# Expert tiles: the hidden rows transposed in 32 by 32 blocks by VectorE and two transfers, in place of TensorE

## The chip, the cores and the metric

The kernel runs on one core of a Trainium2 chip. The number to judge is the time on the device in microseconds, from the start to the end of one execution. TensorE (PE) multiplies matrices, VectorE (DVE), ScalarE (ACT) and GpSimd (POOL) work elementwise, and SyncE (SP) mostly issues transfers. Each engine runs its own list of instructions in order. They meet at semaphores: one engine counts up, another waits for a number.

## The reference

Three layers behind each other, all in fp32: windowed attention, a gated MLP, and a layer of eight experts of which each token uses two. The change lies in the third:

```python
x: (2304, 512)   w1: (8, 512, 1024)   w2: (8, 1024, 512)
top2, top2_w = ...                      # two experts for each token, and their weights
for e in range(E):
    for k in range(2):
        mask = top2[:, k] == e
        h = np.maximum(x[mask] @ w1[e], 0.0)
        out[mask] += top2_w[mask, k, None] * (h @ w2[e])
```

## The kernel before

Tokens are sorted by expert into tiles of 128 rows, `ETILES` = 43 of them; an expert has about five tiles, and the last one or two of the 43 are padding. Products are made in three passes from operands split in two: a high part in TensorE's fp32r format and a low part, the value less the high part (`PRODUCTS`).

One tile t goes through these steps. `load_rows` (SP) brings `x_row`, already with its 32 by 32 blocks moved into place, so that `dve_xT` (VectorE) has only to transpose within blocks (L1801), and then splits the result into `xTh` and `xTl`. `pe_up2` (TensorE) makes x @ w1 in two halves of 512 columns, 12 matmuls each, in banks 0 and 1. `dve_relu` (L1834) writes max(., 0) to `relu` [128 rows, 1024]. `pe_hT` (L1075) transposes `relu` with eight transposes of 128 by 128 into banks 2 and 3. `dve_hT` splits these banks into `hTh` (L1822) and `hTl` (L1824, the bank less `hTh`). `pe_down2` (L1062) makes h @ w2 in 24 matmuls, again in two halves. `dve_y` (L1841) copies the bank to `y_row`, and `store_rows` (SP, L576) stores it; `load_rows` issues at L571.

TensorE's order in the loop is, for tile t: `pe_hT` of t-1, `pe_up2` of t, `pe_down2` of t-1. VectorE's is `dve_hT` of t-1, `dve_relu` of t, `dve_xT` of t+1, `dve_y` of t-1. `hTh`, `hTl` and `relu` exist once; semaphores guard them (`hT_done`, `hTl_done`, `relu_done`, `tile_done`).

Beside that the weights of the next expert but one arrive in 512 KB pieces on ScalarE's queue as soon as an expert's last tile is done. ScalarE casts the high part, and GpSimd makes the low part from two SBUF operands, in two TENSOR_TENSORs of 512 elements for a piece (`expert_piece_low`, L732), eight pieces for an expert. For the last expert's tiles GpSimd gathers finished rows (L750) and adds them (L763), ScalarE scales them, and a last step on VectorE (L1899) follows the last `dve_y`.

## Time and profile before

| | us |
|---|---|
| median of 3 runs | 1078.38 |
| lowest, highest | 1077.81, 1081.57 |
| the profiled execution's own time | 1076.49 |
| its span, on which all rows stand | 1074.7 |
| TensorE busy in it | 1062.6 |
| VectorE busy | 588.3 |
| ScalarE, GpSimd busy | 327.8, 386.8 |

Times in the rows are microseconds from the span's start unless marked ns. A row of a timeline has the start, the length, the engine, the line, the operation, what is written <- what is read, and how many of a kind follow each other (xN, as one length); in brackets stands how long the engine had been idle and what released it. SPq is SP's queue of transfers. A matmul's own length overlaps its neighbours', so the pace is read from starts.

### The profile page before, as it was taken

The page shows a single profiled execution, that of the slowest core. Times are in us where ns is not written, and L with a number is a line of the kernel's source. Part 1 is how long each engine was busy: PE and PEld are TensorE (multiplying, and loading weights), DVE is VectorE, ACT ScalarE, POOL GpSimd, SP SyncE. Part 2 cuts the span into 40 slices and gives each one's busy share as a digit, 9 for nine tenths or more (in the row PEclk, how much of TensorE's full clock was granted, in tenths as well). Part 3 has the DMA queues.
Part 4 walks back from the last instruction along what each step waited for, and adds up shares of the span by engine and source line. Part 5 has one row for each costly group of instructions (what it writes and reads, how often), then busy time and mean ns, then how long its engine had stood idle before and what let it go on. Part 6 is the DMA issues. An engine that isn't in the chain of part 4 may idle for free.

```text
span 1074.7 us, 20097 instructions
## 1 busy us (share of the span) xinstructions
PE 1062.6 (99%) x6053; PEld 931.9 (87%) x6054; DVE 588.3 (55%) x1226; ACT 327.8 (31%) x724; POOL 386.8 (36%) x358
## 2 busy tenths in 40 slices
PE   8999999999999999999999999999999999999998
PEld 7878999999999999999988888888888888888886
DVE  6887434363363463453447775565555556555554
ACT  7987122342342432432352111020302021110222
POOL 4667990030030030120185415070706143250486
PEclk9999999999999999999999999999999999999999
DMA  7985525411311311211074536172616344331676
GB/s 218 276 264 190 176 89 187 127 59 30 118 59 30 117 59 30 98 59 30 26 250 153 161 80 174 39 207 46 195 47 161 85 117 127 82 104 39 168 242 235
DMA packets 199634, 133.18 MB, mean 124 GB/s; under 512 B 128752, under 2 KB 161408, under 8 KB 199584
## 3 DMA queue, kind: packets, MB, share of 16 engines
q1 hardware_dynamic: 177728, 75.14, 25.9%
q10 hardware_dynamic: 16032, 38.47, 10.9%
q0 software_dynamic: 5824, 18.95, 5.1%
q8 instruction: 25, 0.41, 0.2%
q14 instruction: 25, 0.20, 0.1%
HBM read 85.87 MB, written 42.73 MB: 120 GB/s over the span
## 4 chain that ended last, share of the span: by engine, by line
PE 93%; POOL 2%; DMA 2%; issue 1%; DVE 1%; SPq 0%; POOLq 0%; ACT 0%; DVEq 0%
PE bank L873 28%; PE bank L1041 20%; PE bank L1062 20%; PE bank L905 14%; PE bank L1075 3%; PE bank L817 2%; PE bank L844 2%; PE bank L827 1%; POOL token_rows_a L750 1%; PE bank L811 1%; DMA token_rows_b<-expert_rows,slots_u 1%; PE bank L958 1%; DMA q_sb<-in_qT 1%; POOL token_rows_a L763 1%; DMA k_sb<-in_kT 0%
## 5 line engine op out<-in xcount | busy, mean ns | idle before, releaser
L873 PE MATMUL bank<-x_parts,mlp_weights 128*128 128x384 f32 x1704 | 309.4, 336 | 0.0
L873 PEld LDWEIGHTS bank<-x_parts,mlp_weights 128*128 128x128 f32 x1704 | 298.3, 188 | 5.3
L1041 PE MATMUL bank<-expert_parts,xT_high 128*128 (+1 forms) x688 | 216.6, 396 | 0.0
L1062 PE MATMUL bank<-expert_parts,hT_high 128*128 (+1 forms) x688 | 212.2, 390 | 0.0
L732 POOL TENSOR_TENSOR expert_parts<-raw_expert_a,expert_parts 128x512 fp32r<-128x512 f32 x64 | 81.4, 1305 | 234.3 <-ACT expert_parts L1372 232.0
L905 PE MATMUL bank<-mlp_weights,hidden_parts 128*128 128x512 f32 x648 | 162.1, 395 | 0.0
L1062 PEld LDWEIGHTS bank<-expert_parts,hT_high 128*128 128x128 f32 x688 | 129.0, 188 | 26.9 <-issue 0.4
L1041 PEld LDWEIGHTS bank<-expert_parts,xT_high 128*128 128x128 f32 x688 | 125.8, 188 | 24.3 <-issue 0.4
L905 PEld LDWEIGHTS bank<-mlp_weights,hidden_parts 128*128 128x128 f32 x648 | 120.2, 188 | 23.4 <-issue 1.0
L1041 PE MATMUL bank<-expert_parts,xT_low 128*128 (+1 forms) x344 | 134.4, 391 | 0.0
L1062 PE MATMUL bank<-expert_parts,hT_low 128*128 (+1 forms) x344 | 134.2, 390 | 0.0
L1565 DVE TENSOR_TENSOR hidden<-bank,sigmoid 128x384 f32<-128x384 f32 x72 | 40.1, 557 | 139.1 <-ACT sigmoid L1274 138.0
L1372 ACT CAST expert_parts<-raw_expert_a 128x1024 fp32r<-128x1024 f32 x32 | 33.5, 1049 | 262.9 <-PE bank L1062 242.3
L674 POOL TENSOR_TENSOR squares<-squares 128x384 f32<-128x384 f32 x15 | 15.1, 1008 | 251.4 <-ACT squares L1249 251.4
L1834 DVE TENSOR_SCALAR relu<-bank 128x512 f32<-128x512 f32 x86 | 59.0, 690 | 84.0 <-PE bank L1041 84.0
L1841 DVE COPY y_row<-bank 128x512 f32<-128x512 f32 x43 | 29.7, 691 | 108.0 <-PE bank L1062 108.0
L1285 ACT CAST hidden_parts<-hidden 128x384 fp32r<-128x384 f32 x72 | 36.9, 513 | 160.8 <-DVE hidden L1568 154.1
L732 POOL TENSOR_TENSOR expert_parts<-raw_expert_b,expert_parts 128x512 fp32r<-128x512 f32 x64 | 81.1, 1301 | 2.3 <-ACT expert_parts L1372 2.3
L1041 PEld LDWEIGHTS bank<-expert_parts,xT_low 128*128 128x128 f32 x344 | 64.6, 188 | 13.9
L1062 PEld LDWEIGHTS bank<-expert_parts,hT_low 128*128 128x128 f32 x344 | 64.6, 188 | 13.4
L1274 ACT ACTIVATE sigmoid<-bank 128x384 f32<-128x384 f32 x72 | 35.3, 491 | 131.6 <-PE bank L873 130.3
L1571 DVE TENSOR_TENSOR hidden_parts<-hidden,hidden_parts 128x384 fp32r<-128x384 f32 x72 | 47.3, 657 | 46.1 <-ACT hidden_parts L1285 46.1
(220 smaller groups left out, 1230.1 us busy)
## 6 DMA issues: line engine op xcount, KB each, us to landing
raw_expert_a<-in_w ACTq DMA_DIRECT2D x32, 512.0 KB, 4.6
raw_expert_b<-in_w ACTq DMA_DIRECT2D x32, 512.0 KB, 4.2
x_row<-routed_rows SPq DMA_DIRECT2D x172, 64.0 KB, 2.6
expert_rows<-y_row SPq DMA_DIRECT2D x43, 256.0 KB, 2.0
expert_rows<-zeros SPq DMA_DIRECT2D x4, 2304.0 KB, 11.9
v_sb<-in_v SPq DMA_DIRECT2D x32, 256.0 KB, 3.9
q_sb<-in_qT SPq DMA_DIRECT2D x15, 288.0 KB, 3.7
k_sb<-in_kT SPq DMA_DIRECT2D x15, 288.0 KB, 4.1
```

The costliest lines, as they stand in the source:

```text
L732: nc.gpsimd.tensor_tensor(ew_sb[:, slot, 2 * kind + 1, at:at + 512], raw_exp(q)[:, half * 512:half * 512 + 512], ew_sb[:, slot, 2 * kind, ...
L873: last = nc.tensor.matmul(bank[:, 0:CHUNK], w_sb[:, i, wp, at:at + P], xp[:, par, part, k, :], start=n == 0, stop=n == 3 * KB - 1)
L905: last = nc.tensor.matmul(ps[3 + t][:, 0:D], hp[:, i % 2, part, t * P:(t + 1) * P], w_sb[:, i, wp, 2 * KB * P:COLS], start=i == 0 and n == ...
L1041: last = nc.tensor.matmul(ps[half][:, 0:512], (xTh, xTl)[xp][:, buf, k, :], ew_sb[:, bass.ds(slot, 1), wp, k * F2 + half * 512:k * F2 + ha ...
L1062: last = nc.tensor.matmul(y_bank(t)[:, 0:D], (hTh, hTl)[hp][:, f, :], ew_sb[:, bass.ds(slot, 1), 2 + wp, f * D:(f + 1) * D].rearrange("p a ...
L1075: last = nc.tensor.transpose(ps[2 + b][:, f * P:(f + 1) * P], relu[:, col:col + P], ident[:])
L1274: nc.scalar.activation(sig[:], ps[2 * i % 3][:, 0:CHUNK], ACT.Sigmoid).then_inc(sig_done, 1)
L1285: nc.scalar.copy(hp[:, i % 2, 0], h_sb[:]).then_inc(hh_done, 1)
L1372: nc.scalar.copy(ew_sb[:, slot, 2 * kind, piece * 1024:piece * 1024 + 1024], raw_exp(q)).then_inc(expert_high, 1)
L1565: nc.vector.tensor_tensor(h_sb[:], ps[2 * i % 3][:, 0:CHUNK], sig[:], ALU.mult).then_inc(gated, 1)
L1571: nc.vector.tensor_tensor(hp[:, i % 2, 1], h_sb[:], hp[:, i % 2, 0].bitcast(F32), ALU.subtract).then_inc(hl_done, 1)
L1834: nc.vector.tensor_scalar(relu[:, half * 512:half * 512 + 512], ps[half][:], 0.0, None, ALU.max).then_inc(relu_done, 1)
```

## The change

For tiles 4 to 41 the hidden rows are no more transposed by TensorE. VectorE transposes the 32 by 32 blocks straight out of the banks of the layer up (`dve_turn`, to a new buffer `hB`), half by half. SP stores each half to DRAM and loads it back in four pieces with the blocks exchanged, into `relu` (`move_hidden`), each half as soon as it can. `dve_hidden` then takes max(., 0) and splits: the high part in one instruction, the low part in four, all from SBUF. `hB` lies in staging space that is free by then. The last tile and tiles 0 to 3 keep the old way.

```diff
+            def move_hidden(t):
+                for half in range(2):
+                    sp.wait_ge(relu_done, 2 * t + half + 1)
+                    sp.dma_start(hs_dram[t % 2, :, half * 512:half * 512 + 512], hB[:, half * 512:half * 512 + 512]
+                                 ).then_inc(hidden_out[half], 16)
+                for half in range(2):
+                    sp.wait_ge(hidden_out[half], 16 * (t + 1 - FIRST_TURNED))
+
+                    sp.wait_ge(hTl_done, 2 * t - 1 + half)
+                    blocks = hs_dram[t % 2, :, half * 512:half * 512 + 512].rearrange("(s r) (q n) -> q r s n", s=BLOCKS, q=BLOCKS)
+                    for q in range(BLOCKS):
+                        sp.dma_start(relu[q * BLOCK:(q + 1) * BLOCK, half * 512:half * 512 + 512].rearrange(
+                            "r (s n) -> r s n", s=BLOCKS), blocks[q]).then_inc(hidden_in[half], 16)
+
+            for t in range(FIRST_TURNED, ETILES - 3):
+                move_hidden(t)
+                load_rows(t + 3, (t + 3) % 2)
+                store_rows(t - 1)
...
                 now = entries(t)
                 before = entries(t - 1)
-                pe_hT(pe, t - 1)
                 pe_up2(pe, t, buf, *now)
                 pe_down2(pe, t - 1, *before)
...
+        def dve_turn(dve, t, half):
+
+            dve.wait_ge(up_done, 2 * t + half + 1)
+            if not (isinstance(t, int) and t == FIRST_TURNED):
+
+                dve.wait_ge(hidden_out[half], 16 * (t - FIRST_TURNED))
+            nc.vector.transpose(hB[:, half * 512:half * 512 + 512].rearrange("p (q f c) -> p q f c", q=BLOCKS, c=BLOCK),
+                                ps[half][:].rearrange("p (f q c) -> p q f c", q=BLOCKS, c=BLOCK)
+                                ).then_inc(relu_done, 1)
+
+        def dve_hidden(dve, t, halves=(0, 1)):
+
+            dve.wait_ge(tile_done, t)
+            for b in halves:
+                dve.wait_ge(hidden_in[b], 16 * BLOCKS * (t + 1 - FIRST_TURNED))
+                landed = relu[:, b * 512:b * 512 + 512].rearrange("p (s f c) -> p f s c", s=BLOCKS, c=BLOCK)
+                h = hTh[:, 4 * b:4 * b + 4, :].rearrange("p f (s c) -> p f s c", c=BLOCK)
+                nc.vector.tensor_scalar(h, landed, 0.0, None, ALU.max).then_inc(hTh_done, 1)
+                dve.wait_ge(hTh_done, 2 * t + b + 1)
+                low = hTl[:, 4 * b:4 * b + 4, :].rearrange("p f (s c) -> p f s c", c=BLOCK)
+                for s in range(BLOCKS):
+                    last = nc.vector.scalar_tensor_tensor(out=low[:, :, s], in0=landed[:, :, s], scalar=0.0,
+                                                          in1=h[:, :, s].bitcast(F32), op0=ALU.max,
+                                                          op1=ALU.subtract)
+                last.then_inc(hTl_done, 1)
...
             def tile(t, buf, earlier):
-                dve_hT(dve, t - 1)
-                dve_relu(dve, t)
+                dve_turn(dve, t, 0)
+                dve_hidden(dve, t - 1, (0,))
+                dve_turn(dve, t, 1)
+                dve_hidden(dve, t - 1, (1,))
                 dve_xT(dve, t + 1, buf, earlier)
                 dve_y(dve, t - 1)
```

TensorE, where one pass of the loop ends and the next tile begins (L391 and L384 read table entries for the tile, L1064 and L1032 open the layer up). Before:

```order
L1126 COMPARE_AND_BRANCH
L384 TENSOR_LOAD tab
L384 ISA x2
L1075 MATMUL bank<-ident,relu 128x128 [waits hTl_done,relu_done]
L1075 MATMUL bank<-ident,relu 128x128 x3
L1075 MATMUL bank<-ident,relu 128x128 [waits relu_done]
L1075 MATMUL bank<-ident,relu 128x128 x3
L1032 ISA [waits xTl_done]
```

The same place with the change:

```order
L1156 COMPARE_AND_BRANCH
L391 TENSOR_LOAD tab
L391 ISA x2
L1064 ISA [waits xTl_done]
```

The eight transposes are gone and the layer up of the next tile follows at once on the layer down.

VectorE, one tile of its loop. Before:

```order
L1822 CAST hT_high<-bank 128x512 [waits tile_done,hT_done]
L1824 TENSOR_TENSOR hT_low<-bank,hT_high 128x512 [waits hTh_done]
L1834 TENSOR_SCALAR relu<-bank 128x512 [waits hT_done]
L1834 TENSOR_SCALAR relu<-bank 128x512 [waits hT_done,up_done]
L1801 STREAM_TRANSPOSE bank<-x_row 128x512 [waits xTl_done,x_row_in_even]
L1809 CAST xT_high<-bank 128x512 [waits xT_done]
```

With the change (`hidden_blocks` is `hB`; L1876 is `dve_turn`, L1887 and L1891 are `dve_hidden`):

```order
L1876 STREAM_TRANSPOSE hidden_blocks<-bank 128x512 [waits hidden_out_0]
L1887 TENSOR_SCALAR hT_high<-relu 128x512 [waits hidden_in_0]
L1891 SCALAR_TENSOR_TENSOR hT_low<-relu,hT_high 128x4x32 [waits hTh_done]
L1891 SCALAR_TENSOR_TENSOR hT_low<-relu,hT_high 128x4x32 x3
L1876 STREAM_TRANSPOSE hidden_blocks<-bank 128x512 [waits hidden_out_1,up_done]
L1887 TENSOR_SCALAR hT_high<-relu 128x512 [waits hidden_in_1,tile_done]
L1831 STREAM_TRANSPOSE bank<-x_row 128x512 [waits xTl_done,x_row_in_even]
L1839 CAST xT_high<-bank 128x512 [waits xT_done]
```

The split of the tile in front no longer comes ahead of both halves of the layer up. Each half of it stands behind the transpose of a half that the layer up has to finish first.

SP's queue, one tile. Before:

```order
L384 TENSOR_LOAD tab
L571 DMA x_row<-routed_rows 32x16x32
L576 ISA [waits y_row_done]
L576 DMA expert_rows<-y_row 128x512
```

With the change:

```order
L608 DMA hidden_by_blocks<-hidden_blocks 128x512 [waits relu_done] x2
L616 DMA relu<-hidden_by_blocks 32x4x128 [waits hTl_done,hidden_out_0]
L616 DMA relu<-hidden_by_blocks 32x4x128 x3
L616 DMA relu<-hidden_by_blocks 32x4x128 [waits hTl_done,hidden_out_1]
L616 DMA relu<-hidden_by_blocks 32x4x128 x3
L391 TENSOR_LOAD tab [waits xT_done]
L581 DMA x_row<-routed_rows 32x16x32
L586 DMA expert_rows<-y_row 128x512 [waits y_row_done]
```

Ten transfers stand ahead of the load of `x_row`, and the store of `y_row` comes behind them.

## Rows read from the trace of the kernel before

**Rows 1.** The page's busy line, then TensorE's waits: total, times, longest

```profile
PE 1062.6 (99%) x6053; PEld 931.9 (87%) x6054; DVE 588.3 (55%) x1226; ACT 327.8 (31%) x724; POOL 386.8 (36%) x358
...
PE bank L1145 <- DVE ones L1907: 1.3, 1, 1.3
```

**Rows 2.** Timeline of one expert tile: start, length, engine, line

```profile
803.41 1.04 PE L1075 MATMUL bank<-ident,relu 128*128 128x128 f32 x8
...
804.21 0.70 PE L1041 MATMUL bank<-expert_parts,xT_high 128*128 x2
...
804.60 0.36 SPq L576 DMA_DIRECT2D expert_rows<-y_row  x1
...
806.62 3.06 SPq L571 DMA_DIRECT2D x_row<-routed_rows  x4
...
807.35 0.69 DVE L1834 TENSOR_SCALAR relu<-bank 128x512 f32<-128x512 f32 x1 [0.29 <-PE bank L1041]
...
809.55 0.41 PEld L1062 LDWEIGHTS bank<-expert_parts,hT_high 128*128 128x128 f32 x2
809.77 0.62 PE L1062 MATMUL bank<-expert_parts,hT_high 128*128 x2
...
815.22 1.03 PE L1075 MATMUL bank<-ident,relu 128*128 128x128 f32 x8
```

**Rows 3.** VectorE's groups (busy, mean ns), and one timeline row

```profile
L1801 DVE STREAM_TRANSPOSE bank<-x_row 128x512 f32<-128x512 f32 x43 | 30.8, 717 | 0.1
...
L1202 DVE TENSOR_SCALAR qbd<-q_sb 64x576 f32<-64x576 f32 x15 | 11.2, 750 | 0.8
L1492 DVE SCALAR_TENSOR_TENSOR x_chunk<-x_chunk,g_sb,squares 128x384 f32<-128x384 f32 x20 | 11.1, 615 | 0.2
...
239.52 2.21 DVE L1492 SCALAR_TENSOR_TENSOR x_chunk<-x_chunk,g_sb,squares 128x384 f32<-128x384 f32 x4
```

**Rows 4.** L1571: all 72 (ns min/median/max), 11 in 100:170, and timelines

```profile
L1571 DVE TENSOR_TENSOR hidden_parts<-hidden,hidden_parts x72: 557/559/1604, 104.0 to 555.5; 128x384 fp32r<-128x384 f32 x72
...
L1571 DVE TENSOR_TENSOR hidden_parts<-hidden,hidden_parts 128x384 fp32r<-128x384 f32 x11 | 12.7, 1151 | 6.4 <-ACT hidden_parts L1285 6.4
...
103.90 2.86 POOL L611 TENSOR_TENSOR mlp_weights<-raw_mlp,mlp_weights 128x512 fp32r<-128x512 f32 x2
...
104.00 1.60 DVE L1571 TENSOR_TENSOR hidden_parts<-hidden,hidden_parts 128x384 fp32r<-128x384 f32 x1 [0.64 <-ACT hidden_parts L1285]
...
225.73 1.02 POOL L681 TENSOR_TENSOR square_parts<-squares,square_parts 128x384 fp32r<-128x384 f32 x1
225.78 0.98 DVE L1649 TENSOR_SCALAR w_now<-w_now 128x3 f32<-128x3 f32 x1
```

**Rows 5.** GpSimd's splitting (24 such rows from 639 to 955), one VectorE row

```profile
639.76 5.06 POOL L732 TENSOR_TENSOR expert_parts<-raw_expert_a,expert_parts 128x512 fp32r<-128x512 f32 x4 [34.34 <-ACT expert_parts L1372]
...
816.62 5.04 POOL L732 TENSOR_TENSOR expert_parts<-raw_expert_a,expert_parts 128x512 fp32r<-128x512 f32 x4 [38.88 <-ACT expert_parts L1372]
...
949.52 5.03 POOL L732 TENSOR_TENSOR expert_parts<-raw_expert_b,expert_parts 128x512 fp32r<-128x512 f32 x4
...
816.84 0.69 DVE L1824 TENSOR_TENSOR hT_low<-bank,hT_high 128x512 fp32r<-128x512 f32 x1
```

**Rows 6.** Timeline of GpSimd near the end

```profile
1019.61 0.94 POOL L750 DMA_INDIRECT token_rows_a<-expert_rows,slots_u  x1 [4.58 <-DMA expert_rows<-y_row]
...
1026.82 3.79 POOL L763 TENSOR_TENSOR token_rows_a<-token_rows_a 128x512 f32<-128x512 f32 x3
```

**Rows 7.** Stretches (engines' busy, PEclk, DMA share, GB/s); a load's landing

```profile
640.00:660.00 20.00, 20.00 (x94) 16.64 (x93) 12.04 (x18) 7.09 (x7) 19.84 (x16) 1.00 0.87 248
...
6.00:10.00 4.00, 1.95 (x16) 1.63 (x14) 2.13 (x5) 2.53 (x12) 0.63 (x1) 1.00 0.97 308
1070.00:1074.70 4.70, 0.00 (x0) 0.00 (x0) 2.12 (x4) 0.00 (x0) 0.00 (x0) 0.94 0.72 277
...
x_row<-routed_rows SPq DMA_DIRECT2D x172, 64.0 KB, 2.6
```

More of the change, by code:

```diff
@@ L350, in attention_moe_kernel @@
         half_done = sem("half_done")
+        hidden_out = [sem(f"hidden_out_{i}") for i in range(2)]
+        hidden_in = [sem(f"hidden_in_{i}") for i in range(2)]
         y_row_done = sem("y_row_done")
@@ L590, in _ @@
             store_rows(1)
-            with sp.Fori(0, (ETILES - 5) // 2) as m:
-                for a in range(2):
-                    load_rows(2 * m + (5 + a), (5 + a) % 2)
-                    store_rows(2 * m + (2 + a))
-            for t in range(ETILES - 3, ETILES):
-                store_rows(t)
+            load_rows(5, 1)
+            store_rows(2)
+            load_rows(6, 0)
+            def move_hidden(t):
[10 more added lines that the diff above has]
+                            "r (s n) -> r s n", s=BLOCKS), blocks[q]).then_inc(hidden_in[half], 16)
+            assert FIRST_TURNED == 4
+            for t in range(FIRST_TURNED, ETILES - 3):
+                move_hidden(t)
+                load_rows(t + 3, (t + 3) % 2)
+                store_rows(t - 1)
+            for t in range(ETILES - 3, ETILES - 1):
+                move_hidden(t)
+                store_rows(t - 1)
+            store_rows(ETILES - 2)
+            store_rows(ETILES - 1)
             sp.wait_ge(y_row_out, 16 * ONE + 16 * ETILES)
@@ L1114, in tile @@
                 before = entries(t - 1)
-                pe_hT(pe, t - 1)
                 pe_up2(pe, t, buf, *now)
                 pe_down2(pe, t - 1, *before)
-                return now
             fourth = entries(3)
@@ L1128, in pe_experts @@
                 tile(2 * m + 6, 0)
-            before = tile(ETILES - 2, (ETILES - 2) % 2)
             t = ETILES - 1
+            tile(t - 1, (t - 1) % 2)
             now = entries(t)
-            pe_hT(pe, t - 1)
+            before = entries(t - 1)
             pe_up2(pe, t, t % 2, *now)
@@ L1830, in dve_relu @@
                 dve.wait_ge(up_done, 2 * t + half + 1)
-                if not (isinstance(t, int) and t == 0):
+                if isinstance(t, int) and 0 < t < FIRST_TURNED:
                     dve.wait_ge(hT_done, 2 * t - 1 + half)
+                elif isinstance(t, int) and t == ETILES - 1:
+                    dve.wait_ge(hTl_done, 2 * t - 1 + half)
                 nc.vector.tensor_scalar(relu[:, half * 512:half * 512 + 512], ps[half][:], 0.0, None, ALU.max
                                         ).then_inc(relu_done, 1)
+        def dve_turn(dve, t, half):
[19 more added lines that the diff above has]
+                last.then_inc(hTl_done, 1)
         def dve_y(dve, t):
```

22 lines of the change are left out of this document (17 added, 5 removed).

## The prediction

> **What bounds the kernel now.** I read the page's busy line first: TensorE is busy 1062.6 of 1074.7 us. The waits of TensorE come next: the longest in the whole span is 1.3 us [rows 1]. So the end is set by how long TensorE's own instructions take, plus a tail of some 5 us in which the last rows are gathered and written. An instruction taken off TensorE pays in full as long as nobody makes it wait instead.
>
> The timeline of one expert tile gives the lengths [rows 2]. Tiles repeat every 815.22 - 803.41 = 11.81 us. Of that, 24 matmuls of the layer down take 815.22 - 809.77 = 5.45 us, 0.227 us each, and the 24 of the layer up as much again; 10.90 us in all. The other 0.91 us is the eight transposes of `relu` at L1075. VectorE is in nobody's way: it waits 0.29 us for half 0 of the layer up before `relu` starts. What must be watched is how early it has to deliver once its work changes.
>
> **What is removed.** TensorE transposes the hidden rows of tiles 4 to 41 no more: 38 tiles x 0.91 = 34.6 us. All of it lies on the path.
>
> **What is added to VectorE, an ordinary tile.** I count from the first matmul of the layer up of tile t. Half 0 is complete after 12 x 0.227 = 2.72 us; `relu` of before started 807.35 - 804.21 = 3.14 us in, of which 0.11 is the end of the transposes (5.56 us from 804.21 to 809.77, against 5.45). So the new transpose of half 0 starts at 3.03. It costs what L1801 costs, 0.72 us; instructions that don't wait for each other overlap by 0.08 to 0.09 (four L1492 of 0.615 take 2.21), so the next starts 0.63 later, at 3.66 [rows 3]. Then comes half 0 of the split of tile t-1, which before was done at the very start of the tile, on data from TensorE. The high part is one TENSOR_SCALAR from SBUF to SBUF with 512 elements. No such row exists; the nearest is L1202, 0.75 us for 576 elements, so 0.68 us [rows 3]. The low part, one instruction before, is now four SCALAR_TENSOR_TENSORs of 128. L1492, four of 384 in a row, has a spacing of 0.53; with a third of the elements (1.04 ns each) the spacing is 0.27 and the last takes 0.35, together 1.15 us. Half 0 is then split at 3.66 + 0.68 + 0.03 + 1.15 = 5.52. TensorE wants it when it loads the first weights of the layer down, 809.55 - 804.21 - 0.11 = 5.23 us in [rows 2]. It is 0.3 us late. Half 1 (transpose from 5.76, split until 8.25) is wanted at 5.23 + 0.3 + 2.72 = 8.25, just met; the three steps of `dve_xT` end near 10.4 and are wanted near 11.0. So 0.3 us are lost per ordinary tile; the bounds are 0 and 0.6. Ordinary are 32 tiles: +9.6 us (0 to 19).
>
> The Trainium skill (VectorE: DVE Perf Modes, section on Mode 2×_2P) says that a fp32 `tensor_scalar` between SBUF tensors runs two elements a cycle if the outermost counts are even. L1202, with nine blocks, does not show it, and no row here can. By that rule the high part would take an estimated 0.42 us, and the whole sum would come out about 10 us lower.
>
> **What is added in a tile in which GpSimd splits weights.** This is the large term. The new split reads `relu` and `hTh` from SBUF; the old one read a PSUM bank. The trace has rows of VectorE instructions without a PSUM operand beside a GpSimd TENSOR_TENSOR [rows 4]: a TENSOR_SCALAR of three elements, L1649, takes 0.98 us from 225.78 and ends at 226.76, when GpSimd's instruction (225.73 to 226.75) does. L1571, two SBUF inputs, takes 0.56 us when GpSimd rests but 1.15 on average from 100 to 170 us, where GpSimd splits the MLP's weights. At 104.00 it takes 1.60: it waits for the first of two GpSimd instructions, goes next, and the second GpSimd instruction follows it (2.86 for the pair, not 2.52). So such an instruction waits for the running GpSimd instruction, and GpSimd then takes its turn. The split of before, which reads one operand from a PSUM bank, runs its 0.69 us beside GpSimd unhindered (816.84 in [rows 5]).
>
> GpSimd splits an expert's weights in 16 instructions of 1.26 us without a gap, about 20 us, six times between 639 and 955 us, each from 0.6 us after a tile's start [rows 5]. In that tile the ten instructions of the split meet it. The TENSOR_SCALAR waits half of one, 0.63. Each of the four behind it, if turns are taken, has a spacing of 1.26 + 0.04 in place of 0.27: 4 x 1.03 = 4.1. Half 0 is later by 4.75, so TensorE stands still for 5.05. VectorE leaves half 0 at 10.27, transposes half 1 until 10.9, and needs 0.4 + 0.71 + 4.1 + 1.15 more: 17.3. TensorE, done with half 0 at 5.23 + 5.05 + 2.72 = 13.0, waits 4.3 again. The tile loses 9.35 us, lasts 20.2, and GpSimd is through (0.6 + 16 x 1.3 = 21.4) before the next tile's split starts near 23.9. Six tiles: +56 us. The low bound is no waiting at all, 6 x 0.3 = 2; the high one is every one of ten waits in full and exposed, 6 x 12.6 = 76.
>
> **The last tiles.** GpSimd adds gathered rows in groups of three instructions of 1.26 us during tiles 38 to 41 [rows 6]. If a group meets a half it holds it by 0.63 + 2 x 1.03 = 2.7 at most; I take 1.5 for each of four tiles, +6 (0 to 11).
>
> **Transfers.** Each tile adds two stores of 256 KB and eight loads of 64 KB on SP's queue, in front of the load of `x_row` and the store of `y_row`. A store's issue takes 0.36 us and four loads of `x_row` 3.06 [rows 2]; with the same for the new ones SP has 0.72 + at most 6.1 + 3.1 + 0.4 = 10.3 us per tile of 11.2, and likelier 7.2, as the new pieces have fewer, longer runs. Half 0 is stored from 3.75, half 1 from about 6.5; behind that store the four loads of half 0 go out until 8.4 to 9.9 and land 2.6 us later [rows 7], at 11.0 to 12.5. They are read in the next tile, 11.2 + 3.66 = 14.9 after the start: 2.4 to 3.9 us to spare, and as much for half 1, which is one step later on both sides. Hidden, cost 0. The cover is thin where weights arrive (DMA share 0.87 from 640 to 660 us [rows 7]), but there the tile is twice as long. The added register loads on TensorE's sequencer run ahead of the array: 0.
>
> **The sum.** -34.6 + 9.6 + 56 + 6 = +37 us on a span of 1074.7; that run took 1076.5 and the median is 1078.4. Forecast 1078.4 + 37 = **1115 us**, slower.
>
> **Rivals.**
> (B) The four low-part instructions carry no wait between them, and may keep GpSimd out until the last is through. Then a half waits 0.63 + 1.03; the first tile loses 3.0, and the 21 us of splitting reach into a second: 4.5 us per expert, 27 in all. -34.6 + 38 x 0.3 + 27 + 3 = +7: 1085 us, 1074 with a faster TENSOR_SCALAR. For it: no row shows four such instructions in a row beside a busy GpSimd. Against: the turns taken in [rows 4], at 104.00.
> (C) These forms don't wait for GpSimd. Then -34.6 + 11.4 = -23, but the end is GpSimd's: from its gather at 1019.61, which the landing of a `y_row` store released (that of tile 37, five before the last), it works with gaps of 0.3 us on gathers and sums until its last gather lands, 55 us to the end whatever TensorE does [rows 6]. Only 34 transposed tiles lie ahead of that: 34 x 0.61 = 21 us, 1057. This is the one that ends faster. It holds if the held-up time in [rows 4] were due to something else; those rows speak clearly, on L1571's form above all.
> (D) As the forecast, but TensorE's clock drops to 1.2 GHz in the standstills. The rows show a granted clock of 1.00 even from 6 to 10 us, with TensorE busy 1.95 of 4.00, and 0.94 in the stretch after its last matmul [rows 7]; no standstill of 4 to 5 us is in the trace. Priced from rows: the half of down behind the second standstill and the first half of up behind it would take 2.72 us more each, 5.4 per burst, 33 in all: 1148 us. The Trainium skill (TensorE: Matmul & The Clock Gate, section on the HAM clock gate) has the throttled clock as the default that activity releases, which is why this is a rival at all.
>
> **How the numbers follow.** Forecast 0.55, B 0.18, C 0.15, D 0.12. The forecast's own range, from its bounds, is 1090 to 1135; I leave out C and the upper part of D, and take B in: 1074 to 1135. A measurement of this kernel tells about 0.5%, 5.4 us, from no change. Faster by more: C and a little of B, 0.16. Within: half of B, 0.10. Slower: 0.74.
>
> **What would show it.** Right: TensorE's waits on VectorE's `hT_low` come up in six tiles, two of 4 to 5 us each, and of 0.3 us or less elsewhere; the SCALAR_TENSOR_TENSORs there take 1.3 us and 0.35 elsewhere; the removed 0.91 us per tile is gone between experts' splits. If those instructions take 0.35 us beside GpSimd's TENSOR_TENSORs, C is right; if one in four takes 1.3, B; if the granted clock falls below 1.00 behind the waits, D. Waits of TensorE or VectorE that end with a DMA into `relu` would show that the transfers are not hidden, which would make all of this wrong.

## The result and the profile after

The changed kernel takes **1157.81 us** (median of 6 runs, 1155.34 to 1159.57) against 1078.36 us for the kernel before in the same comparison: 1.073 times as long, 95% interval 1.072 to 1.075. It is slower, as forecast, but by 79.5 us, not 37, and outside the range of 1074 to 1135. The profiled execution has a span of 1154.2 us (before: 1074.7). A few executions stood apart from the others of their kernel (one each of e4, 1251 us where the other three took 1232 to 1242, e10, 3754 us, and e11, 2929 us, below), and the ratios leave them out.

Line numbers below are those of the changed kernel: L1073 is the layer up, L1094 the layer down, L1876 VectorE's transposes of the hidden blocks, L1887 the high and L1891 the low part of their split, L1831 to L1841 `dve_xT`, L764 GpSimd's low parts of the weights, L608 and L616 the store and the loads of the hidden blocks, L391 the table loads.

The page's busy line answers to [rows 1]; under it the waits of TensorE (total, times, longest):

```profile
PE 1061.3 (92%) x5749; PEld 909.6 (79%) x5750; DVE 648.3 (56%) x1454; ACT 328.2 (28%) x724; POOL 390.3 (34%) x358
...
PE bank L1094 <- DVE hT_low L1891: 41.5, 15, 4.6
PE bank L1073 <- issue: 32.4, 30, 1.7
PE bank L1073 <- POOL expert_parts L764: 4.8, 4, 1.7
PE bank L1094 <- issue: 2.2, 1, 2.2
```

"issue" means that TensorE stood while it waited for nothing that the profile shows. These two readings account for the whole 79.5 us. TensorE has 304 instructions fewer, yet its busy time fell by 1.3 us only. The 34.6 us of transposes are gone, so the rest has grown by 33.3. Its idle time grew by 92.9 - 12.1 = 80.8 us, and the four rows above sum to 80.9. So: **-34.6** (transposes) **+33.3** (the same matmuls take longer) **+41.5** (waits for the low parts) **+39.4** (gaps of the last three rows).

The 33.3 us have two parts. About 20 us are the clock (an estimate: in stretches of 2 us from 600 us on, the busy time times what the granted clock lacks to 1.00). It is below 1.00 at the six bursts, that is in the tiles in which GpSimd splits weights, and in three places near the end. The other 13 belong to the gaps themselves, at full clock:

```profile
742.40:755.02 12.62, 11.15 (x48) 8.95 (x49) 6.57 (x17) 0.00 (x0) 0.00 (x0) 1.00 0.45 125
```

This stretch is one tile with one gap; TensorE is busy for 11.15 us in it, where the same 48 matmuls took 10.90 without a gap. The last matmul ahead of a gap counts with its whole length (0.39 us, not the 0.227 of the pace), and the first two behind it take 0.72 in place of 0.62. For the 50 gaps of the four rows that is 50 x 0.25 = 12.5 us, so each gap costs 0.25 us more than its idle time.

The gaps of the second row are the surprise. "POOL L764" in the third is the same gap at a burst's end: the layer up waits for the low parts of its own expert's weights, and those were made a burst earlier. The fourth row is another thing, a half that VectorE had ready late among the last tiles. Here is the start of an ordinary tile, in the timeline (start, length, engine, line; in brackets the idle time before), which answers to [rows 2]:

```profile
746.16 0.38 DVE L1887 TENSOR_SCALAR hT_high<-relu 128x512 fp32r<-128x512 f32 x1
...
746.58 0.90 DVE L1891 SCALAR_TENSOR_TENSOR hT_low<-relu,hT_high 128x128 fp32r<-128x128 f32 x4
...
749.21 0.90 DVE L1891 SCALAR_TENSOR_TENSOR hT_low<-relu,hT_high 128x128 fp32r<-128x128 f32 x4
...
751.50 0.69 DVE L1841 TENSOR_TENSOR xT_low<-bank,xT_high 128x512 fp32r<-128x512 f32 x1
...
755.02 0.72 PE L1073 MATMUL bank<-expert_parts,xT_high 128*128 x2 [1.47 <-issue]
```

VectorE is not late in this tile. Half 1 of the low parts is there at 750.11, just in time; the next `xT_low` at 752.19; and still TensorE stands for 1.47 us before 755.02 (in every second tile, where the loop's branch does not stand ahead as well, for 0.81). What it does in that time is in the rows of TensorE's sequencer, which are not timed as busy (window 748 to 757: count, ns min/median/max, first and last start):

```profile
L391 PEldq FUSED_REGOPS  x7: 46/151/151, 752.1 to 754.3; - x7
L391 PEldq TENSOR_LOAD <-tab x4: 297/300/301, 751.6 to 753.9; - x4
L391 PEldq SEQ_ASSERT  x4: 18/18/18, 752.3 to 754.5; - x4
```

Four loads from the table, each with its register arithmetic 0.72 us, run from 751.6 to 754.5; the next tile's matmuls can only be issued behind them. In the trace of the kernel before (window 803 to 815) the same four stand here:

```profile
L384 PEldq TENSOR_LOAD <-tab x4: 297/300/307, 811.3 to 813.3; - x4
```

They start 3.9 us before the array is through with its tile at 815.22 [rows 2], and lie hidden.

The second of the six bursts, in the timeline (it answers to [rows 5]):

```profile
709.32 0.72 PE L1073 MATMUL bank<-expert_parts,xT_high 128*128 x2 [0.81 <-issue]
...
709.74 5.25 POOL L764 TENSOR_TENSOR expert_parts<-raw_expert_a,expert_parts 128x512 fp32r<-128x512 f32 x4 [50.56 <-ACT expert_parts L1402]
...
713.12 0.70 DVE L1887 TENSOR_SCALAR hT_high<-relu 128x512 fp32r<-128x512 f32 x1
...
713.86 5.08 DVE L1891 SCALAR_TENSOR_TENSOR hT_low<-relu,hT_high 128x128 fp32r<-128x128 f32 x4
...
719.10 1.22 PE L1094 MATMUL bank<-expert_parts,hT_high 128*128 x2 [4.03 <-DVE hT_low L1891]
...
720.39 5.11 DVE L1891 SCALAR_TENSOR_TENSOR hT_low<-relu,hT_high 128x128 fp32r<-128x128 f32 x4
...
725.65 0.73 PE L1094 MATMUL bank<-expert_parts,hT_high 128*128 x2 [1.06 <-DVE hT_low L1891]
...
730.39 0.73 PE L1073 MATMUL bank<-expert_parts,xT_high 128*128 x2 [1.72 <-POOL expert_parts L764]
```

Four low-part instructions take 5.08 us beside GpSimd and 0.90 when it rests. The tile lasts 730.39 - 709.32 = 21.07 us. The second wait is only 1.06 us long, since TensorE was slow in between: without the lower clock its twelve matmuls would have been done 2.8 us earlier. The same burst in stretches (engines' busy time, then the granted clock, DMA share, GB/s; it answers to [rows 7]):

```profile
709.30:719.10 9.80, 5.75 (x24) 4.45 (x25) 6.61 (x8) 4.43 (x5) 9.36 (x8) 0.94 0.82 247
719.10:722.00 2.90, 2.90 (x7) 2.35 (x8) 2.87 (x4) 1.17 (x2) 2.90 (x3) 0.50 0.90 275
722.00:725.60 3.60, 2.59 (x7) 1.49 (x5) 3.60 (x4) 1.04 (x1) 3.60 (x4) 0.62 0.94 307
725.60:730.40 4.80, 3.04 (x13) 2.20 (x13) 2.61 (x4) 1.06 (x1) 4.77 (x4) 1.00 0.79 269
```

The granted clock falls to 0.50, that is 1.2 GHz, near 718, still within the standstill of 4 us, and is back at 1.00 near 724.5. All twelve matmuls of the half in between run at it.

### The profile page after: what moved, and what is told of

Read it like the earlier page. It is cut to its first block, busy times and chain, and to the rows that moved or that the text cites. A ratio compares the mean times of both kernels' runs of the same rounds, so it can differ in the third digit from the quotient of the medians.

```text
span 1154.2 us, 19963 instructions
## 1 busy us (share of the span) xinstructions
PE 1061.3 (92%) x5749; PEld 909.6 (79%) x5750; DVE 648.3 (56%) x1454; ACT 328.2 (28%) x724; POOL 390.3 (34%) x358
## 4 chain that ended last, share of the span: by engine, by line
PE 54%; issue 29%; POOL 10%; DVE 3%; DMA 2%; SPq 1%; ACT 0%; DVEq 0%; POOLq 0%; ACTq 0%
PE bank L905 24%; PE bank L937 12%; POOL expert_parts L764 10%; PE bank L1094 6%; PE bank L1073 5%; PE bank L849 2%; PE bank L876 2%; PE bank L859 1%; PE bank L843 1%; DMA k_sb<-in_kT 1%; DVE hT_low L1891 1%; DMA routed_rows<-y_sb,slot_now 1%; PE bank L990 1%; DMA x_row<-routed_rows 1%; POOL routed_rows L728 0%
## 5 line engine op out<-in xcount | busy, mean ns | idle before, releaser
L1094 PE MATMUL bank<-expert_parts,hT_high 128*128 (+1 forms) x688 | 228.3, 415 | 43.8 <-DVE hT_low L1891 41.5
L1073 PE MATMUL bank<-expert_parts,xT_high 128*128 (+1 forms) x688 | 216.8, 396 | 37.2 <-issue 32.4
L1094 PEld LDWEIGHTS bank<-expert_parts,hT_high 128*128 128x128 f32 x688 | 136.9, 201 | 80.1 <-issue 51.3
L1073 PEld LDWEIGHTS bank<-expert_parts,xT_high 128*128 128x128 f32 x688 | 126.4, 188 | 76.5 <-issue 52.2
L764 POOL TENSOR_TENSOR expert_parts<-raw_expert_a,expert_parts 128x512 fp32r<-128x512 f32 x64 | 83.6, 1339 | 289.6 <-ACT expert_parts L1402 287.2
L1094 PE MATMUL bank<-expert_parts,hT_low 128*128 (+1 forms) x344 | 141.4, 411 | 0.0
L1073 PE MATMUL bank<-expert_parts,xT_low 128*128 (+1 forms) x344 | 134.3, 391 | 0.0
L1876 DVE STREAM_TRANSPOSE hidden_blocks<-bank 128x512 f32<-128x512 f32 x76 | 54.3, 715 | 139.4 <-PE bank L1073 135.2
L1891 DVE SCALAR_TENSOR_TENSOR hT_low<-relu,hT_high 128x128 fp32r<-128x128 f32 x304 | 124.9, 472 | 2.6
L764 POOL TENSOR_TENSOR expert_parts<-raw_expert_b,expert_parts 128x512 fp32r<-128x512 f32 x64 | 82.2, 1316 | 1.7 <-ACT expert_parts L1402 1.7
L1094 PEld LDWEIGHTS bank<-expert_parts,hT_low 128*128 128x128 f32 x344 | 68.9, 200 | 15.1
L1073 PEld LDWEIGHTS bank<-expert_parts,xT_low 128*128 128x128 f32 x344 | 64.6, 188 | 13.3
```

What stands on the lines that cost most here:

```text
L764: nc.gpsimd.tensor_tensor(ew_sb[:, slot, 2 * kind + 1, at:at + 512], raw_exp(q)[:, half * 512:half * 512 + 512], ew_sb[:, slot, 2 * kind, ...
L1073: last = nc.tensor.matmul(ps[half][:, 0:512], (xTh, xTl)[xp][:, buf, k, :], ew_sb[:, bass.ds(slot, 1), wp, k * F2 + half * 512:k * F2 + ha ...
L1094: last = nc.tensor.matmul(y_bank(t)[:, 0:D], (hTh, hTl)[hp][:, f, :], ew_sb[:, bass.ds(slot, 1), 2 + wp, f * D:(f + 1) * D].rearrange("p a ...
L1876: nc.vector.transpose(hB[:, half * 512:half * 512 + 512].rearrange("p (q f c) -> p q f c", q=BLOCKS, c=BLOCK), ps[half][:].rearrange("p (f ...
L1891: last = nc.vector.scalar_tensor_tensor(out=low[:, :, s], in0=landed[:, :, s], scalar=0.0, in1=h[:, :, s].bitcast(F32), op0=ALU.max, op1=A ...
```

## The experiments

**Theory 1**: the table loads lie open, because half 1 is released so late that the sequencer has no lead left over the array. **Theory 2**: GpSimd and VectorE's instructions with two SBUF inputs take turns, instruction by instruction. Rivals: the gaps or the bursts belong to transfers, to the x rows, or to the clock alone. All times are medians; the kernel before, run beside them, took 1076 to 1079 us, and the changed kernel takes 1158.

### Theory 1: the gap ahead of the up layers

**e1**, the loads moved (the first tile's layer up is taken out ahead of the loop):

```diff
-                now = entries(t)
-                before = entries(t - 1)
-                pe_up2(pe, t, buf, *now)
-                pe_down2(pe, t - 1, *before)
+                before = entries(t - 2)
+                now = entries(t)
+                pe_down2(pe, t - 2, *before)
+                pe_up2(pe, t, buf, *now)
```

> The changed kernel with one edit on TensorE's side: the four table loads of a tile stand between its up layer and the down layer of the tile before, not ahead of the up layer, so that the sequencer does them while the array still has the up layer's matmuls. Theory 1 (the loads, 0.72 us each from 751.6 to 754.5, lie open since half 1 of the low parts comes late and the sequencer has no lead left): the gap of 1.47 us ahead of each up layer goes, ordinary tiles fall from 12.3-12.6 to about 11.1 us, the time by 35 to 45 us, to about 1118. Rival (the gap belongs to a transfer, to the x rows or to VectorE): no change, 1158. Under both the six bursts stay as they are, with STT groups of four at 5 us.

**e2**, VectorE's order turned round:

```diff
-                dve_turn(dve, t, 0)
                 dve_hidden(dve, t - 1, (0,))
-                dve_turn(dve, t, 1)
+                dve_turn(dve, t, 0)
                 dve_hidden(dve, t - 1, (1,))
+                dve_turn(dve, t, 1)
```

> The changed kernel with VectorE's order turned round in the loop: half 0 of the hidden layer is split before half 0 of the next tile is transposed, half 1 before half 1. Theory 1 (what lies open is the time from the release of half 1 to the next up layer's first matmul, 4.9 us, of which the sequencer's loads are 2.9): half 1 is released about 2 us earlier in ordinary tiles, the gap of 1.47 us closes without any change on TensorE's side, 30 to 45 us less, about 1120. Rival (the loads would show wherever they stand, or the gap is another's): within 5 us of 1158. A third way: the transposes come later, the hidden loads land too late for the next split, and the tile grows: over 1165.

**e4**, one line more ahead of the tile's loads:

```diff
+                entries(t - 2)
                 now = entries(t)
```

> The changed kernel with two more table loads ahead of each up layer in the loop (their values are not used). Theory 1: the gap ahead of the up layer grows by 2 x 0.72 = 1.45 us in each of 37 tiles, 1.47 to 2.9 us, 45 to 54 us more, about 1208. Rival (the sequencer's loads are hidden and the gap is another's): within 5 us of 1158.

**e10**, the control on the kernel before:

```diff
+                entry(pe, t + T_SLOT, 1)
                 now = entries(t)
                 before = entries(t - 1)
                 pe_hT(pe, t - 1)
```

> The kernel before with a fifth table load ahead of each tile in TensorE's loop (its value is not used). Theory 1: its sequencer starts the loads 3.9 us before the array is through with the down layer (811.3 against 815.2) and has them done at 813.9; one more, 0.72 us, is still covered: at most 5 us more, 1078 to 1083. Rival (a load costs its time wherever it stands): 37 x 0.72 = 27 us more, 1105; in the changed kernel the same dose cost that much (two loads more, 54 us more of waits).

Measured: e1 **1113.7** us (44 less), e2 **1109.7** (48 less), e4 **1238.4** (81 more), e10 **1080.9** (ratio to before 1.004, 1.002 to 1.006). TensorE's waits of e1:

```profile
PE bank L1094 <- DVE hT_low L1894: 39.6, 16, 3.9
```

Of e2:

```profile
PE bank L1094 <- DVE hT_low L1891: 23.4, 10, 3.5
PE bank L1073 <- issue: 10.3, 9, 2.1
PE bank L1073 <- POOL expert_parts L764: 4.8, 3, 2.6
```

Of e4:

```profile
PE bank L1073 <- issue: 82.5, 35, 3.4
PE bank L1094 <- DVE hT_low L1892: 36.0, 13, 4.8
PE bank L1073 <- POOL expert_parts L764: 9.0, 3, 3.1
```

In e1 the gaps ahead of L1073 are gone and the waits for VectorE are nearly as they were. The 44 us are about what the 34 gaps cost, 37.2 idle and 34 x 0.25. e2 touches nothing on TensorE's side and yet brings the gaps from 37.2 to 15.1 us, and the waits for half 1 from 41.5 to 23.4; that loads cost their time wherever they stand does not explain it. In e4 they grew from 37.2 to 91.5 us, 54 us for two loads more in 37 tiles: 0.73 us a load, as their rows say. That the time grew by 81 is the clock again: its profiled execution, with a span of 1249 us, shows TensorE busy for 45 us more with the same matmuls, and by the same estimate as above the clock takes 65 us of it in place of 20. I had not counted that in. The same kind of load costs the kernel before next to nothing (4.7 us for 37), since its sequencer has a lead. Theory 1 stands.

### Theory 2: the bursts

**e3**, GpSimd's low parts cut short (n is 512, and 8 from the second pair of experts on; the rest of these low parts is left out); **e8**, in smaller pieces, with the semaphore raised by every second one; **e14**, the transfers of the weights alone cut to 64 columns from the second pair on (most of these weights are left out). The three edits in this order:

```diff
-                                            ew_sb[:, slot, 2 * kind, at:at + 512].bitcast(F32), ALU.subtract
+                                            ew_sb[:, slot, 2 * kind, at:at + n].bitcast(F32), ALU.subtract
...
-                    expert_piece_low(pair, q)
+                    expert_piece_low(pair, q, 8)
```
```diff
-                for half in range(2):
-                    at = piece * 1024 + half * 512
+                for half in range(4):
+                    at = piece * 1024 + half * 256
```
```diff
+            if not isinstance(pair, int):
+                dst, src = (dst[..., 0:64], src[..., 0:64])
             act.dma_start(dst, src).then_inc(expert_in[q % 4], 16)
```

> The changed kernel in which GpSimd's low parts of the experts' weights cover 8 columns of each 512 from the second pair of experts on (the rest of these low parts is left out; instructions, waits and transfers keep their number). Theory 2 (the bursts cost what they do because GpSimd's and VectorE's two-input instructions take turns at the memory): STT groups of four take 0.90 us everywhere, the waits of 4.0, 1.1 and 1.7 us at each burst go, the granted clock stays at 1.00 behind them, 52 to 62 us less, about 1100. Rival (the weights' transfers or the casts on ScalarE, which stay, make the bursts): 0 to 10 us less. Theory 1 holds as before: the gaps ahead of the up layers stay, some 1.3 us a tile.

> The changed kernel with GpSimd's low parts in pieces of 256 columns instead of 512, twice as many. Theory 2 (turns are taken by whole instructions: each of VectorE's four waits for one of GpSimd's): the STT group of four falls from 5.1 us to about 3, the stall of a burst by half, 20 to 28 us less, about 1133. Rival (the two engines share the bandwidth evenly, so that the number of bytes counts and not the length of a piece): groups of four stay near 5 us, within 5 us of 1158, or slower by GpSimd's fixed cost per instruction.

> The changed kernel in which only the transfers of the experts' weights are cut to 64 columns of 512 or 1024 from the second pair on (so these weights are mostly left out); GpSimd's and ScalarE's instructions keep their size. Theory 2: the bursts stay, groups of four STT at 5 us, waits of 4 us and more for half 1: at most 15 us less, 1143 to 1158. Theory 3 as the main cause of the bursts in this kernel too: 35 to 60 us less, under 1123.

Measured: e3 **1113.0** us (45 less; 52 to 62 expected), e8 **1135.3** (23 less, as expected), e14 **1157.6** (no change). TensorE's waits of e3:

```profile
PE bank L1073 <- issue: 33.9, 30, 1.8
PE bank L1094 <- DVE hT_low L1891: 7.6, 5, 2.1
```

A burst of e8 in the timeline, VectorE's and GpSimd's rows:

```profile
710.43 2.92 DVE L1892 SCALAR_TENSOR_TENSOR hT_low<-relu,hT_high 128x128 fp32r<-128x128 f32 x4
...
712.44 6.11 POOL L764 TENSOR_TENSOR expert_parts<-raw_expert_b,expert_parts 128x256 fp32r<-128x256 f32 x8
```

With GpSimd's pieces half as long, the same four instructions of VectorE take 2.92 us in place of 5.08, beside the same bytes: it is the length of the piece in front that each waits for, and no sharing of bandwidth. Part of e8's 23 us is the clock, which stays at 1.00 in all its bursts, where the waits are shorter, and its busy line shows the cost of the gaps bare:

```profile
PE 1046.0 (93%) x5749; PEld 897.1 (79%) x5750; DVE 628.0 (56%) x1454; ACT 328.2 (29%) x724; POOL 410.9 (36%) x486
```

At a mean granted clock of 0.998, TensorE is still busy for 18 us more than 1062.6 - 34.6 = 1028.0, with some 60 gaps in it. The gaps of theory 1 are not smaller in e3 (33.9 and 6.9 us). e14 takes away most of the weights' transfers beside a burst and leaves 41.2 us of waits, as before: in this kernel these transfers cost nothing.

e3 fell short of its expectation. It wins about 34 us of waits and 15 of clock, and its gaps are 3.6 us longer; the 7.6 us of waits that were left I had not foreseen. The next runs show what such waits belong to.

### A third cost behind the two

**e5** has e1 and e2 together, **e6** e1 and e3, **e11** the edits of e1, e3 and e14 (e6 and e11 leave out what e3 and e14 do), and **e7** does the split through the PSUM banks that TensorE's transposes used, with the orders of e5:

```diff
-                nc.vector.tensor_scalar(h, landed, 0.0, None, ALU.max).then_inc(hTh_done, 1)
+                nc.vector.tensor_scalar(bank.rearrange("p f (s c) -> p f s c", c=BLOCK), landed, 0.0, None, ALU.max
+                                        ).then_inc(bank_filled, 1)
+                dve.wait_ge(bank_filled, 2 * t + b + 1 - 2 * FIRST_TURNED)
+                nc.vector.tensor_copy(hTh[:, 4 * b:4 * b + 4, :], bank).then_inc(hTh_done, 1)
...
-                for s in range(BLOCKS):
-                    last = nc.vector.scalar_tensor_tensor(out=low[:, :, s], in0=landed[:, :, s], scalar=0.0,
+                nc.vector.tensor_tensor(hTl[:, 4 * b:4 * b + 4, :], bank,
```

> The changed kernel with both edits, the table loads between the up layer and the down layer, and VectorE's split ahead of its transpose. Theory 1: both edits close the same gap (44 and 48 us each when alone), so they don't add up; what the second adds is the waits that the first left (10 us ahead of the up layers, 39.6 against 23.4 us for half 1): 1095 to 1102. If each edit had removed a cost of its own, the sum would be 1066. What is left are the bursts alone.

> The changed kernel with the table loads between the layers and GpSimd's low parts cut to 8 columns of 512 from the second pair on (the rest of these low parts is left out). Theories 1 and 2 together: two separate costs, 44 and 45 us when taken away one at a time, so both away give 1158 - 89 = 1069 (1064 to 1074), below the kernel before, as taking out the transposes alone would have been. If a third cost of the new path lies behind them (transfers, VectorE late in ordinary tiles), the time stays above 1078.

> The changed kernel with both edits of the order, and the hidden layer split by way of the PSUM banks that the transposes used: VectorE writes the rectified blocks into a bank, and cast and difference read that bank as in the kernel before, so that no VectorE instruction of the split has two inputs in SBUF. It computes all of the reference. Theory 2 (only instructions with two SBUF inputs take turns with GpSimd): the bursts cost nothing, VectorE has 1.5 us more work a tile inside a tile of 10.9 us, and the time is that of before less the transposes: 1045 to 1060. Rival (any SBUF input or output of VectorE takes turns with GpSimd): the bursts still cost 5 to 9 us each, 1080 to 1105.

> The kernel of e6 (table loads between the layers, GpSimd's low parts 8 columns of 512) in which also the transfers of the experts' weights are cut to 64 columns of 512 or 1024 from the second pair on (so these weights are mostly left out; instructions and waits keep their number). Theory 3 (the third cost is the hidden blocks' round trip beside these transfers): the store lands in about 2 us everywhere, the waits of 25 us go and the clock stays at 1.00, 1045 to 1058. Rival (the third cost is SyncE's own queue, full at a tile of 10.9 us, or VectorE): the waits stay at over 15 us, 1080 to 1095.

Measured: e5 **1101.9** us, e6 **1092.4**, e7 **1093.0**, e11 **1056.3** (ratio to before 0.981, 0.979 to 0.983). e5 overlaps as theory 1 says. e6 misses the sum of the two costs, 1069, by 23 us, and e7 its forecast by over 30. Their traces show where the time went. This is the second burst of e7:

```profile
704.81 1.92 SPq L609 DMA_DIRECT2D hidden_by_blocks<-hidden_blocks  x2
...
709.97 3.64 SPq L617 DMA_DIRECT2D relu<-hidden_by_blocks  x8
...
716.23 0.69 DVE L1891 TENSOR_SCALAR bank<-relu 128x512 f32<-128x512 f32 x1 [5.54 <-DMA relu<-hidden_by_blocks]
...
718.53 1.22 PE L1095 MATMUL bank<-expert_parts,hT_high 128*128 x2 [3.23 <-DVE hT_low L1896]
```

The SCALAR_TENSOR_TENSORs are gone, and with them the turns. Now SyncE stands 3.2 us for the store's landing (706.73 to 709.97), VectorE 5.5 us for the loads, TensorE 3.2 us for VectorE. SyncE's waits for the store from 600 us on, of e6:

```profile
SPq L616 <- DMA hidden_by_blocks<-hidden_blocks: 55.3, 23, 5.8
```

The same of e11:

```profile
SPq L616 <- DMA hidden_by_blocks<-hidden_blocks: 19.7, 23, 3.6
```

Without the weights' transfers beside it the store lands sooner, TensorE's waits for the low parts are 5.3 us in all, and the clock costs little, some 3 us: TensorE is busy for 1032.1 us, which is the 1062.6 of before less 34.6, within 4. The same cut of the transfers is worth 36 us here and nothing in e14. In this kernel the time of a transfer costs only where nothing else is late.

Four of the next five runs were meant to shorten this path and so to beat the kernel before. **e9** loads the x rows while half 0 lands; **e12** paces the weights over three tiles, **e13** does that to the changed kernel alone; **e15** puts the four pieces of each half on the store's side and leaves one load, and **e16** is e15 with the pacing of e12. The edits of e9, of e12 and e13, and of e15:

```diff
+                    if half == 0:
+                        between()
+                    sp.wait_ge(hidden_out[half], 16 * (t + 1 - FIRST_TURNED))
...
-                move_hidden(t)
-                load_rows(t + 3, (t + 3) % 2)
+                move_hidden(t, lambda: load_rows(t + 2, t % 2))
```
```diff
-            if q % 8 == 0:
+            if q % 8 == 0 or (q % 8 in (2, 4) and not isinstance(pair, int)):
...
-                    act.wait_ge(tile_done, entry(act, 2 * pair + (T_END + slot - 2), 64))
+                    act.wait_ge(tile_done, entry(act, 2 * pair + (T_END + slot - 2), 64) + q % 8 // 2)
```
```diff
-                    sp.dma_start(hs_dram[t % 2, :, half * 512:half * 512 + 512], hB[:, half * 512:half * 512 + 512]
-                                 ).then_inc(hidden_out[half], 16)
+                    for s in range(BLOCKS):
+                        sp.dma_start(blocks[s], hB[s * BLOCK:(s + 1) * BLOCK, half * 512:half * 512 + 512].rearrange(
+                            "r (q n) -> r q n", q=BLOCKS)).then_inc(hidden_out[half], 16)
```

> The kernel of e7 with SyncE's queue in another order: the x rows of the tile after next are loaded while the first half's store lands, and each half is loaded back behind its own store, where e7 issued both stores, stood 2 to 6 us for them and came to the loads after that. It computes all of the reference. Theory 3 (what e6 and e7 have left, 25 and 30 us of waits for half 1 or half 0, is the round trip of the hidden blocks, lengthened to 6 us from store to load where the next experts' weights are transferred): half 0 starts its way back about 2 us earlier, the waits of 29.6 us fall to about 10, 1065 to 1078. Rival (the round trip's landing times alone set it, whatever the order): 1088 to 1098.

> The kernel of e7 in which ScalarE starts an expert's next weights two pieces at a time, the second pair of pieces a tile later than the first and the rest two tiles later, instead of all eight at once. It computes all of the reference for these inputs (five or six tiles an expert). Theory 3: the transfers and GpSimd's work are spread over three tiles, the hidden blocks' store lands in about 3 us instead of 6, the waits of 29.6 us fall under 10 and the clock stays at 1.00: 1055 to 1068. Rival (the round trip is late by SyncE's own queue): 1085 to 1095.

> The changed kernel with the same pacing and nothing else. Theory 2 (each of VectorE's two-input instructions that meets GpSimd waits for one of its instructions, and a tile has only 0.3 us of slack): the number of meetings is nearly kept, so little is won, 1140 to 1158. Rival (most of a burst's cost is the round trip beside the transfers, or GpSimd's unbroken run): under 1120.

> The kernel of e7 with the blocks rearranged by the store instead of the load: four stores of 32 partitions for each half, issued right behind its transpose, and one load of 128 partitions for each half, with the x rows' loads between the two loads. The transfers move the same blocks, and SyncE issues as many as before. Theory 3 (what is left of the new path's cost is the length of the round trip): the issue time of the four transfers lies ahead of the store's landing, where half 1 still has to be transposed, not behind it; the hidden halves are back 2 to 3 us earlier, most of the 29.6 us of waits goes, 1060 to 1072. Rival (the landing times beside the weights' transfers set it, or scattered stores land later than plain ones): 1085 to 1100.

> The same kernel with the weights paced as in e12. Theory 3: e12 had 21.6 us of waits left, which the shorter round trip covers: 1050 to 1062, the first below the kernel before by over 1.5%. Rival: as for e15, within 5 us of e12's 1088.

Measured: e9 **1113.5**, e12 **1087.7** (ratio 1.009, 1.007 to 1.010), e13 **1140.5**, e15 **1130.1**, e16 **1135.0** us. e13 came out at the lower edge of what theory 2 has. The other four missed. I had looked at the landing times and not at SyncE's own queue, which works in order through waits and issues; what follows is read from their traces, and no further run tests it. SyncE's waits of e9 from 600 us on:

```profile
SPq L617 <- DMA hidden_by_blocks<-hidden_blocks: 109.0, 44, 7.2
```

The same of e12:

```profile
SPq L617 <- DMA hidden_by_blocks<-hidden_blocks: 57.2, 35, 4.6
```

The eight stores of one tile of e15 in the timeline, the single ones of this tile and its neighbours (ns min/median/max), and SyncE's waits for VectorE in the tile (us, times, longest):

```profile
750.89 6.59 SPq L611 DMA_DIRECT2D hidden_by_blocks<-hidden_blocks  x8
...
L611 SPq DMA_DIRECT2D hidden_by_blocks<-hidden_blocks x24: 303/433/500, 739.8 to 775.6; - x24
...
SPq L611 <- DVE hidden_blocks L1881: 3.3, 3, 2.9
```

e9 makes SyncE stand for each half's store by itself, 109 us in all where e7 stood 58.2. In e12 the weights are spread out, but SyncE stands for the stores as long as in e7. In e15 and e16 the waits for the stores are nearly gone (7.2 and 7.4 us), but SyncE now stands 142 and 150 us for VectorE, and VectorE 143 and 139 us for the loads. The eight stores are not slow to issue: one takes 0.43 us, as a load of the same size does in e7, and 2.9 of the 6.59 us are the wait for half 1's transpose. The tile is as long as a circle through both engines. In e15 SyncE issues the load of half 1 at 749.62; VectorE can split that half at 752.93 and has transposed the next half 1 by 755.69; SyncE issues four stores until 757.48, then the load of half 0, a table load and the x rows until 761.66, and only then, at 761.76, the next load of half 1. That is 12.1 us, where TensorE would need 10.9.

e12 is the best that computes the whole reference (its pacing counts on five or six tiles for each expert, as these inputs have), and it is still 9 us behind the kernel before. No variant that computes everything beats the kernel before. That the transfers could be moved to a less busy queue was not tried.

## Why the prediction was wrong, step by step

- **Removed, -34.6 us: right.** e11 shows it bare: with nothing in the way TensorE is busy 30.5 us less than before.
- **"The added register loads on TensorE's sequencer run ahead of the array: 0": wrong, and the largest miss**: 37.2 us of gaps, some 46 with the 0.25 us that each costs besides, and e1 gets 44 back. This is the step that failed. Four loads a tile stand in both kernels, so they are not even added; what changed is their cover. In the kernel before, the sequencer had the last low parts early; its loads started about 3.9 us before the array was through (811.3 against 815.22), and took 2.6. In the changed kernel it must wait for half 1 until 750.11, issues what is left by 751.6, and loads until 754.5, while the array runs dry at 753.55. I asked whether VectorE met the array's deadline and took "just met" as free. The sequencer's deadline is about 1.5 us earlier (an estimate: the length of the gap).
- **An ordinary tile's split late by 0.3 us, +9.6: wrong in size, to the other side.** The TENSOR_SCALAR takes 0.38 us, not 0.68, and the four low parts 0.90, not 1.15, so VectorE is in time in the ordinary tiles but the first (1.2 us); each costs its gap instead. Here the Trainium skill (VectorE: DVE Perf Modes, section on Mode 2×_2P) had the better figure: two elements a cycle for a one-source instruction between SBUF tensors, an estimated 0.42 us. The trace agrees. I had set it aside for the row of L1202, which has an odd number of blocks.
- **Bursts, turns at the memory: right in mechanism**, with 5.08 us for the four low parts where 1.15 + 4.1 was put. Of the 9.35 us of standing forecast per burst 5.1 are there in this one (4.03 and 1.06); 2.8 of the rest went into slow matmuls. That the tile's 21.07 us come close to the forecast 20.2 is in part luck, as 2.8 us of clock and the gap of 1.72 at its end stand where more waiting was forecast. The twelve waits of the six bursts come to 35.3 us, where the forecast had 56. The Trainium skill (SBUF — State Buffer, section on the two separate sides) calls the shared port pair an exclusive lock held for the whole instruction. e8 agrees: the wait goes with the length of GpSimd's piece.
- **Rival D, the clock: it was no rival but part of the result**, and a term that the forecast put at nothing. Its price of 33 us was too high: the clock cost about 20, as the lower clock did not last over two halves in each burst. That TensorE's busy time rose by 33.3 us is a coincidence, since 13 of them belong to the gaps. I gave D 0.12 since no row showed a standstill of this length. The forecast plus D was 1148.
- **Rivals B and C: wrong.** The four instructions do not keep GpSimd out (5.08 us, not 1.7), and they do wait.
- **The last tiles, +6: about right.** Three waits of 0.6, 2.2 and 4.4 us come to 7.2. Before the longest the turns show again, with GpSimd's sums in place of its splits:

```profile
1129.55 5.05 DVE L1891 SCALAR_TENSOR_TENSOR hT_low<-relu,hT_high 128x128 fp32r<-128x128 f32 x4
...
1130.55 3.69 POOL L795 TENSOR_TENSOR token_rows_a<-token_rows_a 128x512 f32<-128x512 f32 x3
```

- **Transfers hidden, 0: right for this kernel**: VectorE waits once for them, 3.4 us near the end, and the weights' transfers beside them cost nothing (e14). "The cover is thin where weights arrive, but there the tile is twice as long" was true, and it is why e6 and e7 fell short: as soon as the tile is no longer twice as long, the cover is gone.

From the forecast +37 to the measured +79.5 the terms go, as estimates with 0.25 us for each gap: the loads +46, the clock +20, the bursts -18, the ordinary tiles -8, the last tiles +2. That is 42 of 42.5 us. The error would have been larger had the bursts and the ordinary tiles not come out cheaper.

The signs of right and wrong that the prediction named did appear. Waits of TensorE for `hT_low` came in groups at the bursts, and the clock fell behind them. The kind "issue" was on no list.

## What to carry to other kernels

An engine has two deadlines: the array's and that of its sequencer, which must get through its register loads and issues before the array runs dry. When a change makes a producer deliver later, look at what stands in the sequencer's stream behind the wait (here 2.9 us of table loads), and put such loads ahead of the wait, under work that is already queued. Price a standstill of TensorE of a few microseconds with the slow matmuls behind it, and don't add up the gains of removed costs: the next latest thing, here SyncE's queue with its waits for landings, takes its share. Don't put a rise of busy time down to the clock before the granted clock says so; gaps lengthen it as well. And a timeline row of several instructions can hold a wait.

## What the hardware showed

- A table load on TensorE's sequencer costs 0.72 us with its register arithmetic (0.30 for the load, 0.15 for a FUSED_REGOPS); e4 measures 0.73 as a slope. It is nearly free with a lead (e10: 4.7 us for 37) and costs its full time without.
- A gap of TensorE costs 0.25 us beyond its idle time at full clock (11.15 us busy in a tile with one gap, 10.90 without).
- The granted clock fell to 1.2 GHz within a standstill of 4 us that came after 5.75 us of work, and came back some 6 us later. It stayed at 1.00 in the tiles with gaps of 1.5 and 0.8 us by turns (1.00 from 742.4 to 755.0 us), and in the bursts of e8, where the waits are shorter. In e4, with gaps of about 2.1 and 3.0 us by turns, it fell again and again, and TensorE's busy time rose by another 45 us.
- The two engines take turns, instruction by instruction: four VectorE instructions beside GpSimd pieces of 1.3 us take 5.08 us, beside pieces of 0.76 (half as many elements) 2.92, alone 0.90.
- The issue of a DMA of 64 KB on SyncE's queue takes 0.43 us (median), from DRAM into 32 partitions (e7) and from 32 partitions to DRAM (e15) alike.
